# Queries and keys with the head dimension in partitions from the start, in a top-k attention and two-block kernel on one core

## The reference

```
scores = scale * q @ k.T                      # per batch and head, 576 x 576
kth    = 32nd largest of each row
attn   = softmax(where(scores >= kth, scores, -1e9))
x      = (attn @ v), heads side by side       # 1152 x 512
x      = ((x @ w_a) * (x @ w_b)) @ w_out      # 512 -> 1536 -> 512
out    = sum over e of p[:, e] * (relu(x @ w1[e]) @ w2[e])   # 512 -> 1024 -> 512
```

## Time and profile before

| | |
|---|---|
| median of 3 runs | 821.5 us (820.43 to 822.25) |
| profiled execution | 819.9 us, of it 818.1 us span |
| mean granted clock of PE | 0.981 of full speed |
| DMA | 80710 packets, 97.94 MB, mean 120 GB/s |
| chain that ended last | PE 81%, DVE 7%, ACT 5%, POOL 3% |

### The profile page before, as it was taken

How to read it: one execution, slowest core, us unless ns; L and a number is a source line. 1 busy time by engine, 2 the same in 40 slices (tenths; PEclk the granted TensorE clock), 3 DMA queues, 4 the chain that set the end, 5 groups by cost and what they waited for, 6 DMA issues and landing times.

```text
span 818.1 us, 14224 instructions
## 1 busy us (share of the span) xinstructions
PE 776.1 (95%) x5141; PEld 683.6 (84%) x5141; DVE 574.8 (70%) x1147; ACT 436.0 (53%) x848; POOL 356.0 (44%) x322
## 2 busy tenths in 40 slices
PE   4468999999999999999999999999999999999998
PEld 3347878888888888888988898999898999989997
DVE  5999999989999999999346853563456444464423
ACT  6687777787777777777664432342134322343210
POOL 2868774444455554545334302562135521464100
PEclk9588999999999999999999999999999999999999
DMA  9450684466545484445578001300032002220101
GB/s 242 130 156 6 240 289 143 155 205 189 181 156 180 137 280 154 150 150 173 183 261 263 18 26 53 103 26 0 26 104 78 1 1 78 63 67 1 52 1 65
DMA packets 80710, 97.94 MB, mean 120 GB/s; under 512 B 32896, under 2 KB 60032, under 8 KB 80640
## 3 DMA queue, kind: packets, MB, share of 16 engines
q1 hardware_dynamic: 79584, 96.77, 37.5%
q10 hardware_dynamic: 1056, 0.26, 0.2%
HBM read 86.00 MB, written 11.01 MB: 119 GB/s over the span
## 4 chain that ended last, share of the span: by engine, by line
PE 81%; DVE 7%; ACT 5%; POOL 3%; issue 3%; DMA 0%; ACTq 0%; SPq 0%; POOLq 0%; DVEq 0%
PE ps L801 24%; PE ps L733 21%; PE ps L638 15%; PE ps L623 8%; PE ps L551 4%; PE ps L587 4%; PE ps L564 3%; DVE m L1131 2%; PE ps L596 2%; DVE work L1137 2%; POOL p_sb L1363 1%; DVE work L1125 1%; POOL h_sb L1382 1%; DVE m L1121 1%; ACT s_sb L873 1%
## 5 line engine op out<-in xcount | busy, mean ns | idle before, releaser
L1131 DVE MAX8 m<-work 128x8 f32<-128x576 f32 x216 | 152.4, 748 | 0.0
L733 PE MATMUL ps<-x_hi,w_hi 128*128 128x256 f32 (+1 forms) x448 | 132.8, 296 | 0.7 <-DVE u_sb L1244 0.4
L801 PE MATMUL ps<-w_lo,h_hi 128*128 128x512 f32 x288 | 112.8, 392 | 0.0
L801 PE MATMUL ps<-w_hi,h_lo 128*128 128x512 f32 x288 | 112.7, 391 | 0.0
L801 PE MATMUL ps<-w_hi,h_hi 128*128 128x512 f32 x288 | 112.6, 391 | 0.0
L1363 POOL TENSOR_TENSOR p_sb<-s_sb,p_sb 128x576 f32<-128x576 f32 x72 | 101.8, 1431 | 19.0 <-ACT p_sb L879 18.5
L1137 DVE MATCH_REPLACE8 work<-m,work 128x576 f32<-128x576 f32 x144 | 106.0, 744 | 0.0
L1435 POOL TENSOR_TENSOR u_sb<-u_sb,p_sb 128x256 f32<-128x256 f32 (+1 forms) x32 | 31.6, 988 | 161.9 <-DVE u_sb L1257 161.9
L1264 DVE TENSOR_TENSOR c_sb<-ps,p_sb 128x256 f32<-128x256 f32 (+1 forms) x32 | 14.7, 458 | 119.1 <-PE ps L733 119.0
L733 PEld LDWEIGHTS ps<-x_hi,w_hi 128*128 128x128 f32 x448 | 84.5, 189 | 2.4 <-DVE u_sb L1244 0.6
L991 ACT ACTIVATE h_hi<-c_sb 128x256 fp32r<-128x256 f32 (+1 forms) x32 | 14.2, 444 | 120.7 <-DVE c_sb L1264 120.7
(11 more groups left out here) (125 smaller groups left out, 2023.1 us busy)
## 6 DMA issues: line engine op xcount, KB each, us to landing
wo<-wo_d SPq DMA_DIRECT2D x96, 512.0 KB, 5.0
w_raw<-moe_w_in SPq DMA_DIRECT2D x32, 256.0 KB, 3.3
w_raw<-moe_w_in SPq DMA_DIRECT2D x16, 512.0 KB, 4.8
wo_d<-wo SPq DMA_DIRECT2D x12, 512.0 KB, 4.9
w_raw<-moe_w_a_in SPq DMA_DIRECT2D x4, 768.0 KB, 5.2
w_raw<-moe_w_b_in SPq DMA_DIRECT2D x4, 768.0 KB, 4.9
wo_raw<-moe_w_out_in SPq DMA_DIRECT2D x12, 256.0 KB, 3.7
x_d<-x_out_sb SPq DMA_DIRECT2D x9, 256.0 KB, 2.9
```

The costliest lines, as they stand in the source:

```text
L733: mm = nc.tensor.matmul(ps[:, bank, 0:NH[g]], w, x, start=first and c == n == 0, stop=last and c == HK - 1 and n == 2, skip_group_check=True)
L801: mm = nc.tensor.matmul(ps[:, DOWN_BANKS[j], 0:DM], h[:, f, tok], w[:, f, :], start=m == f == n == 0, stop=m == FM - 1 and f == 1 and n == 2)
L1131: nc.vector.max(m8[:, par, i, 8 * r:8 * r + 8], work[:, i, :]).then_inc(ve_top, 1)
```

## The change

kernel() lays out the inputs before the launch: q as (tile, 128 = two heads x 64, pair, token), k as (batch, pair, 128, 576) with the odd head rotated by 64, v as (batch, token, 512), and each slice of w_a and w_b contiguous per partition. Only moves of numbers are made there. In the program:

- all transposes of keys and queries and their copies go, and SP or ACT loads kT and qT directly; SP loads a tile's queries once the scores that read the buffer are done;
- PE does eight matmuls on zeros (WARM) ahead of scores(0); DVE's first two max read the banks, and ACT's copies of scores(0) follow them;
- slices and chunks move between slots; in slot 5 ACT and POOL do the first tile's high and low part ahead of the softmax work; slice 7's high part comes behind inv_out;
- the second batch's keys are loaded by one DMA in slot 10, its values in slot 11; the zeros in v_sb[1] are written at the start;
- w1_high(1) on ACT and w2_low(0) on POOL move from slot 40 behind the last unit.

The diff, cut to its core:

```diff
+        WARM = 8
-        HIGH_IN = {0: (0, 1, 2), 1: (3,), 2: (4,), 3: (5,), 4: (6, 7)}
-        LOW_IN = {0: (0, 1), 1: (2,), 2: (3,), 3: (4,), 4: (5,), 5: (6, 7)}
-        CHUNKS_IN = {6: (0, 1, 2, 3), 7: (4, 5), 8: (6, 7, 8), 9: (9, 10, 11)}
+        HIGH_IN = {0: (0, 1), 1: (2, 3), 2: (4, 5), 3: (6,), 4: (7,)}
+        LOW_IN = {0: (0,), 1: (1, 2), 2: (3, 4), 3: (5,), 4: (6,), 5: (7,)}
+        CHUNKS_IN = {6: (0, 1, 2), 7: (3, 4, 5), 8: (6, 7, 8), 9: (9, 10, 11)}
...
+                sp.dma_start(qT[:, t % 2, :, :], q[t]).then_inc(ld_q[t % 2], 16)
...
+                sp.dma_start(kT[:, 0, pr, :], k[0, pr]).then_inc(ld_k[pr], 16)
...
+            load_k(0)
+            load_k(1)
+            load_slice(0)
+            load_k(2)
+            load_slice(1)
+            load_k(3)
+            load_slice(2)
+            load_v(0)
             load_q(1)
-            load_v(0)
...
+                if n and n % PR == 0 and n // PR + 1 < NT:
+                    sp.wait_ge(pe_s, n)
+                    load_q(n // PR + 1)
+                if n == 10:
+                    sp.wait_ge(po_wo, FO)
+                    sp.dma_start(kT[:, 1, :, :], k[1].rearrange("r p s -> p r s")).then_inc(ld_k1, 16)
+                if n == 11:
                     load_v(1)
...
+            pe.wait_ge(ve_z, 1)
+            for i in range(WARM):
+                nc.tensor.matmul(ps_b[:, 0:P], x_inv[:].rearrange("p r h -> p (r h)"), x_inv[:].rearrange("p r h -> p (r h)"),
+                                 start=True, stop=True)
+            scores(0)
             pe.wait_ge(po_id, 2)
-            keys_pair(0, 0)
...
-            for pr in range(1, PR):
-                keys_pair(0, pr)
...
+                if n == 0:
+                    act.wait_ge(ve_top, head + 1)
...
+                if scaled_tile(n) == 0:
+                    x_hi(0)
                 if j is not None:
                     below_top(j, 0)
...
-                if n == NP + 4:
-                    w1_high_raws(1)
-                    w1_high_sums(1)
...
+                for i in HIGH_IN.get(n, ())[0:1]:
+                    if n == 1:
+                        slice_hi(i)
...
                 for i in HIGH_IN.get(n, ()):
-                    slice_hi(i)
+                    if n < PR and (n, i) != (1, 2):
+                        slice_hi(i)
...
-                if next_q(n) is not None:
-                    q_out(next_q(n), 0, PR, ps_a)
                 if scaled_tile(n + 1) is not None:
                     inv_out(scaled_tile(n + 1))
...
+                if n == PR:
+                    slice_hi(7)
             h_out(NP - 1)
+            w1_high_raws(1)
+            w1_high_sums(1)
             p1_out(0)
...
+                    if n == 0:
+                        dve.wait_ge(pe_s, 1)
+                        nc.vector.max(m8[:, par, i, 0:8], ps_sc[i]).then_inc(ve_top, 1)
...
                 if j is not None:
-                    push_down(j, 0)
                     if scaled_tile(n) == 0:
                         x_low(0)
+                    push_down(j, 0)
                     push_down(j, 1)
...
             product(NP - 1)
             hidden_low(NP - 1)
+            w2_low(0)
```

More of the change, by code:

```diff
@@ L714, in _ @@
                     inv_spread(scaled_tile(n + 1))
-                if n in KEYS1:
-                    pe.wait_ge(ac_pT, 2 * pair_of(n) + 2)
-                for part in KEYS1.get(n, ()):
-                    if part == "tail":
-                        pe.wait_ge(ld_kt[1], 16)
-                        keys_tail(1, range(PR))
-                    else:
-                        keys_pair(1, part)
                 if pair_of(n) is not None:
@@ L1083, in _ @@
                     copy(b_sb[:], ps_b[:, 0:FS], ACT.Copy).then_inc(ac_b, 1)
-                if next_q(n) is not None:
-                    q_out(next_q(n), 0, PR, ps_a)
                 if scaled_tile(n + 1) is not None:
                     inv_out(scaled_tile(n + 1))
-                for part in KEYS1.get(n, ()):
-                    if part == "tail":
-                        keys_tail(1, 0, PR, KEYS0 + 1)
-                    else:
-                        keys_pair(1, part)
+                if n == PR:
+                    slice_hi(7)
             h_out(NP - 1)
+            w1_high_raws(1)
+            w1_high_sums(1)
             p1_out(0)
@@ L1352, in _ @@
             pool.wait_ge(po_pick, PR + 1)
+            for side in range(2):
+                nc.gpsimd.memset(other_half(1, side), 0.0).then_inc(po_z, 1)
+                pool.wait_ge(po_z, side + 1)
             def limits(n):
@@ L1460 @@
     nc = bacc.Bacc("TRN2", target_bir_lowering=False, num_devices=1)
+    b, h, s, d = inputs["q"].shape
+    pairs, half = h // 2, s % P
+    laid = dict(inputs)
+    turned = inputs["q"].reshape(b, pairs, 2, s, d).transpose(1, 2, 4, 0, 3).reshape(pairs, P, b * s // P, P)
+    laid["q"] = turned.transpose(2, 1, 0, 3)
+    turned = inputs["k"].reshape(b, pairs, 2, s, d).transpose(0, 1, 2, 4, 3)
+    laid["k"] = np.concatenate([turned[:, :, 0], np.roll(turned[:, :, 1], half, axis=-1)], axis=2)
+    laid["v"] = inputs["v"].transpose(0, 2, 1, 3).reshape(b, s, h * d)
+    for name in ("moe_w_a", "moe_w_b"):
+        dm, ff = inputs[name].shape
+        laid[name] = inputs[name].reshape(dm // P, P, pairs, ff // pairs).transpose(2, 1, 0, 3)
     arrays, args = {}, []
     for name in INPUTS:
-        a = np.ascontiguousarray(inputs[name])
+        a = np.ascontiguousarray(laid[name])
         arrays[name + "_in"] = a
         args.append(nc.dram_tensor(name + "_in", a.shape, F32, kind="ExternalInput").ap())
-    b, h, s, d = inputs["q"].shape
     out = nc.dram_tensor("out", (b * s, h * d), F32, kind="ExternalOutput").ap()
-    ff = inputs["moe_w_a"].shape[1]
-    dm = inputs["moe_w_a"].shape[0]
     wo_d = nc.dram_tensor("wo_d", (ff // P, P, 2 * dm), F32, kind="Internal").ap()
     x2_d = nc.dram_tensor("x2_d", (dm, b * s), F32, kind="Internal").ap()
-    build(nc, *args, wo_d, x2_d, out)
+    build(nc, (b, h, s, d), *args, wo_d, x2_d, out)
     return run(nc, [arrays], core_ids=[0]).results[0]["out"]
```

196 lines of the change are left out of this document (33 added, 163 removed).

## The result

The changed kernel takes **818.8 us** (median of 10 runs, 818.2 to 819.7) against 821.5 for the one before (820.4 to 822.3): a ratio of 0.9968, with a 95% interval of 0.9958 to 0.9978. That is 2.7 us faster. The forecast was 813.8, range 808.5 to 817.5. It is faster, as said, but by a third of what was summed, and outside the range.

A forecast was written before the change was run, and what follows sets the result against it. PE's work, plus time it isn't fed, was taken to bound the kernel, with DVE pacing the start and POOL slots 6 to 9. -4.3 - 3.2 - 2.7 + 2.5 = -7.7 us from 821.5 gave 813.8, range 808.5 to 817.5.

The forecast's parts named there:

- Step 1: Start of the kernel: without transposes ahead of the first scores, DVE starts 3.3 us earlier.
- Step 2: Slots 1 to 5: POOL about 1 us late, PE's first weight product 3.9 us earlier, first h_sb 4.3 us earlier.
- rival (b): Start: POOL's lateness over slots 1 to 3 grows to 3 us, first product gains under 1; 817.1 us, chance 0.12.
- Step 3: Slots 6 to 9: POOL is the bound and the chunk count is unchanged, so 44.97 us stay; 0.
- Steps 4 and 5: Slots 10 to 14 lose key transposes and copy waits, -3.2 us; six PE-bound slots lose query transposes, -2.7 us.
- Step 6: End of first block: moved high and low parts make PE wait, DVE and POOL collide; +2.5 us.
- Rival (d): PE's clock stays at 1.2 GHz through slots 5 to 7; about 832 us, chance 0.03.

The follow-up runs named there:

- t_early: Changed kernel with a one-column activation ahead of ScalarE's first copy of scores, so the table load comes early; 815.76 us, ratio 0.9933.
- s_before: Changed kernel with the weight slices placed as in the kernel before, all else as changed; 815.5 us, ratio 0.9929.
- b_slices: Kernel before the change with the weight slices placed as in the changed kernel, nothing else changed; 824.29 us, ratio 1.0034.
- w_w1back: Changed kernel with only ScalarE's rounding of the second w1 group back in the first block's last slot; 814.65 us, ratio 0.9917.
- w_w2back: Changed kernel with only GpSimd's low part of w2 back in the first block's last slot; 814.91 us, ratio 0.9924.
- c_w2: Changed kernel with slices placed as before, early table load and GpSimd's w2_low back in the last slot; 812.44 us, ratio 0.9885.
- s_warm0: s_before without the 8 warming matmuls on TensorE (WARM = 0); 816.32 us, ratio 0.9935.

## Why the prediction was wrong

**Step 1, the start**, forecast -3.3 on DVE: the first max came 3.5 us earlier, the second pair only 1.93. "The copies that follow a max fit under the other head's max" was right for the copies (0.19 us of wait in t_early), but the table load in front of the first of them was left out: 1.28 us. In the earlier trace rows it doesn't show, since ACT did it at 1.81 us, when nothing else could be done. And the forecast looked at DVE alone: scores(1), which feed ACT's and POOL's slices, were not in it, and took 2.29 us.

**Step 2, weight slices and the first tile**, is where it failed: the first product was forecast 3.9 us earlier (59.5) and came 0.3 us earlier (63.10). "POOL falls behind by about 1 us" and "the sums wait about 0.5 us": it fell behind by 4.8 us, and the sums waited 3.00. The limits of three pairs in a row start 10.82 and 12.57 us apart, not 10.2. Left out of the sum were POOL's wait of 0.89 us for ACT between limits and subtraction for each of these pairs, 1.67 us in slot 2 for ACT's high part, which stands behind p_out, which waits 0.99 us for PE's transposes at half clock, and 0.7 us that slot 0 already lay behind. Part of this is the half clock, by these rows: in the kernel before, with these transposes at full speed (0.63 us for four, 1.09 here), ACT's wait in slot 2 was 0.43, and with scores(1) at 1.24 us POOL's first low part would have ended before DVE's first pair did. That makes about 1.3 of the 4.8 us, an estimate; no run kept the clock up at the start. A slot's length on an engine was made from its busy time and not from its chain. s_before and b_slices show it from both sides: -3.0 and, less the 1.0 that is not the placement, +3.5 us on the start of DVE's sums. So rival (b) came true for the start (first product -0.3, first h_sb -1.0 instead of -4.3), by the lateness of 3 us and more that it names; I gave it 0.12.

**Step 3, chunks**, 0: right as to the chunks (44.94 against 44.91). But "44.97 us stay" was wrong, it took 46.65, because POOL is the bound only as long as DVE is ahead. In slot 9 DVE paces, 0.26 us late at its sums and 0.82 at its scaling, as above. With the lead restored the slots take 44.91.

**Steps 4 and 5**: slots 10 to 14 52.93 us against 52.9 forecast; four-slot periods 41.87 against 41.8.

**Step 6, the way out**, +2.5: PE's two waits and the collision came as worked out. From send(34) the loss is 439.60 - 425.18 = 14.42 us against 10.69 before (440.96 - 430.27): +3.7. The 1.2 us over are the granted clock after the waits, 1.5 us on send(35), which no term held, less 0.3 by which the rest was shorter. In two of six profiles that clock did not fall, so this part differs from execution to execution. Rival (d) put the danger of the clock at the start. Its form did not come, 0.50 through slots 5 to 7 (1.00 from 70 us on), but the clock was at 0.50 from 10 to 50 us, before the stretch that (d) reckons with, and by the rows that was part of the lateness of step 2.

In sum, on the profiled executions: -1.0 at the first h_sb and +1.7 in slots 6 to 9, together +0.65 where -4.3 was forecast; -5.7 from there to send(34), forecast -5.9 (right in size and by the mechanism that was summed, though no run took these two changes back); +3.7 on the way out, forecast +2.5. That makes -1.4 where -7.7 was forecast: 5.0 us of the miss lie at the start and in slots 6 to 9 and 1.2 on the way out. The medians of the runs have -2.7.

## What to carry to other kernels

Before work is moved onto an engine that others wait for, write its chain for the slot with every wait in it, not its busy time, and ask how late it is at each step that releases another engine: lateness adds from slot to slot. A new wait ahead of an engine's first job can push back something that is done with that job, such as a table load. And two instructions of VectorE and GpSimd that slow each other are worth parting by a single move; moving both together keeps them together.

## What the runs showed of the hardware

- DVE and GpSimd, subtracting between SBUF operands at the same time, take turns by whole instructions. In the changed kernel DVE's raw part runs from 429.64 for 1.23 us, as long as alone. POOL's w2_low is given from 429.71 for 3.39 us: 1.1 until DVE's part ends, and 2.3, its own length of 2.38 to 2.41. DVE's sum part is given from 430.78 for 3.14: 2.3 until POOL's ends, and 0.8, about its own 0.95. The Trainium skill ("SBUF — State Buffer", "Who interferes with whom") says that they lock each other out, and the rows agree. It hits small instructions too: DVE's sum over 8 columns (x_den) took 0.72 us in slot 9, beside a POOL row from 99.16 to 100.16, and ended with that row at 100.19; so did it in t_early (0.71 us) and w_w1back (0.66). Elsewhere it took 0.14 to 0.18 us. It has one SBUF input where the subtractions have two; what makes it wait isn't shown.
- The granted clock fell to 0.50 in the stretch behind two waits of 0.77 and 1.95 us in four of six profiles, twice not. It did not fall behind a wait of 0.77 alone (w_w2back, c_w2, one profile each). The longer one alone was not tried.
- The granted clock that the profile reports isn't always the speed at which matmuls ran. In s_warm0 it is 1.00 in 10 to 20 us, and the eight matmuls of scores take 2.29 us there, as at 0.50, and 1.24 at full speed later (b_slices has 1.00 up to 30 us and scores of 2.29 us in it, too):

```profile
10.00:20.00 10.00, 4.46 (x16) 2.39 (x16) 10.00 (x23) 5.31 (x5) 5.07 (x2) 1.00 0.62 209
```

```profile
13.54 2.29 PE L492 MATMUL ps<-kT,qT 64*128 64x288 f32 x8 [1.37 <-ACT s_sb L764]
...
45.75 1.24 PE L492 MATMUL ps<-kT,qT 64*128 64x288 f32 x8 [0.79 <-ACT pT L788]
```

So the mean clock of that kernel, 0.990 against 0.977 for s_before, says nothing of a faster start.
